# Taking two attention accumulators out of PSUM: one VectorE copy of 576 columns against one copy each by VectorE and ScalarE

## What is computed

```python
q_pool = q.reshape(B, H, S // 2, 2, D).mean(axis=3)
scores = scale * np.matmul(q_pool, k.transpose(0, 1, 3, 2))
attn = np.exp(scores - max(scores)); attn = attn / (sum(attn) + 1e-09)
x = np.matmul(attn, v)                       # -> (2304, 512)
h = x @ w_in;  x = (h * sigmoid(h)) @ w_out          # d_ff 2048
a = x @ w1; b = x @ w2; out = ((a * b) @ w3) @ w_out2
```

## Time and profile before

| | us |
|---|---|
| median of 3 runs | 1280.03 |
| lowest and highest | 1279.23, 1280.61 |
| the profiled execution | 1280.76 |
| its span, first to last instruction | 1278.6 |

### The profile page before, as it was taken

One profiled execution on the slowest core, in us unless ns is written; L12 is line 12 of the kernel. 1 busy time (PEld: TensorE's weight loads), 2 busy tenths in 40 slices (PEclk: granted clock), 3 DMA queues, 4 the chain that ended last, 5 costly groups with the idle time before them and its releaser, 6 DMA issues.

```text
span 1278.6 us, 26209 instructions
## 1 busy us (share of the span) xinstructions
PE 1268.6 (99%) x10968; PEld 1148.6 (90%) x10968; DVE 601.3 (47%) x895; ACT 587.6 (46%) x1065; POOL 378.1 (30%) x321
## 2 busy tenths in 40 slices
PE   8999999999999999999999999999999999999998
PEld 7999999999999999888888888888988888888888
DVE  6778877777787778723212121111155222222222
ACT  3777777777777777833222222222245212121111
POOL 5577777777777776210000000000000000000000
PEclk9999999999999999999999999999999999999999
DMA  4222222222222211021000000001062000000001
GB/s 143 66 75 73 66 73 72 74 76 75 75 75 75 75 57 38 27 68 50 9 1 1 1 1 1 1 1 50 1 207 74 1 26 8 10 24 1 33 8 42
DMA packets 26005, 58.59 MB, mean 46 GB/s; under 512 B 7200, under 2 KB 8736, under 8 KB 25888
## 3 DMA queue, kind: packets, MB, share of 16 engines
q1 hardware_dynamic: 25888, 56.91, 13.4%
HBM read 52.04 MB, written 4.79 MB: 44 GB/s over the span
## 4 chain that ended last, share of the span: by engine, by line
PE 97%; DVE 2%; DMA 0%; ACT 0%; issue 0%; DVEq 0%; ACTq 0%
PE psum L957 19%; PE psum L958 19%; PE psum L959 19%; PE psum L1035 18%; PE psum L974 10%; PE psum L1010 9%; PE psum L1012 3%; DVE mx L745 1%; PE psum L985 1%; DMA qraw<-in_qT 0%; DVE pL L780 0%; ACT pH L566 0%; PE psum L1045 0%; ACT tmpB L559 0%; ACT pF L574 0%
## 5 line engine op out<-in xcount | busy, mean ns | idle before, releaser
L745 DVE TENSOR_REDUCE mx<-psum 128x2 f32<-128x768 f32 x240 | 229.0, 958 | 85.3 <-PE psum L974 82.1
L566 ACT ACTIVATE pH<-psum 128x576 fp32r<-128x576 f32 x288 | 188.5, 655 | 133.9 <-PE psum L1012 129.1
L471 POOL TENSOR_TENSOR pL<-pF,pH 128x576 fp32r<-128x576 f32 x120 | 170.2, 1428 | 111.6 <-ACT pF L574 111.4
L888 DVE TENSOR_TENSOR gL<-gF,gH 128x512 fp32r<-128x512 f32 (+1 forms) x80 | 51.1, 639 | 310.2 <-ACT gH L647 310.2
L1035 PE MATMUL psum<-pH,vH 64*128 64x288 f32 x1152 | 180.5, 295 | 0.9 <-ACT tmpB L559 0.5
L1035 PE MATMUL psum<-pL,vH 64*128 64x288 f32 x1152 | 178.6, 292 | 0.8 <-DVE pL L780 0.8
L1035 PE MATMUL psum<-pH,vL 64*128 64x288 f32 x1152 | 178.5, 292 | 0.0
L644 ACT ACTIVATE gF<-psum 128x512 f32<-128x512 f32 (+1 forms) x80 | 44.4, 555 | 269.9 <-PE psum L959 269.9
L935 DVE TENSOR_TENSOR pr<-aS,psum 128x512 f32<-128x512 f32 (+1 forms) x40 | 25.4, 635 | 200.2 <-ACT aS L716 200.2
L1035 PEld LDWEIGHTS psum<-pH,vH 64*128 64x128 f32 x1152 | 117.0, 185 | 2.4 <-PE psum L1035 1.6
L957 PE MATMUL psum<-gH,woH 128*128 128x512 f32 (+1 forms) x320 | 117.9, 368 | 0.0
(11 more groups left out here) (104 smaller groups left out, 2762.5 us busy)
## 6 DMA issues: line engine op xcount, KB each, us to landing
vraw<-in_v SPq DMA_DIRECT2D x16, 576.0 KB, 4.5
qraw<-in_qT SPq DMA_DIRECT2D x15, 576.0 KB, 5.5
kraw<-in_kT SPq DMA_DIRECT2D x15, 576.0 KB, 3.7
rsums<-recips SPq DMA_DIRECT2D x32, 144.0 KB, 3.0
wstage<-in_w_in SPq DMA_DIRECT2D x16, 256.0 KB, 4.1
fstage<-in_w3T SPq DMA_DIRECT2D x8, 512.0 KB, 4.4
w12stage<-in_w SPq DMA_DIRECT2D x8, 512.0 KB, 4.7
outT<-oS SPq DMA_DIRECT2D x4, 1024.0 KB, 4.2
```

What stands on the lines that cost most here:

```text
L471: pool.tensor_tensor(pL[r][:], pF[SLOT[n]][:], pH[r][:].bitcast(F32), ALU.subtract).then_inc(pL_pool, 1)
L566: act.activation(pH[r][:], scores, ACT.Exp, scale=SCALE).then_inc(pH_ready, 1)
L745: dve.tensor_reduce(mx[:, qt, :, kb], bank[:, :, 0:KW], AX.X, ALU.max).then_inc(max_taken, 1)
L888: dve.tensor_tensor(gL[r][:, w], gF[:, w], gH[r][:, w].bitcast(F32), ALU.subtract).then_inc(gL_ready, 1)
```

## The change

One VectorE instruction copies both accumulators, 2 x 288 = 576 columns from two banks, at VectorE's old place in the order; ScalarE's copies are gone. A tensor `outs` with room for both heads takes the place of `tmpA` and `tmpB`, in the same bytes of SBUF. `o_taken` counts one for each half.

```diff
-        tmpA, tmpB = [None, sb("tmpA1", [2, HALF])], [None, sb("tmpB1", [2, HALF])]
+        outs = [None, sb("outs1", [2, 2, HALF])]
...
-                sp.wait_ge(o_taken, 4 * (p + 1))
-                for tmp, row, into in ((tmpA[p % 2], D, 0), (tmpB[p % 2], 0, 1)):
+                sp.wait_ge(o_taken, 2 * (p + 1))
+                for hd, row, into in ((0, D, 0), (1, 0, 1)):
...
-            def take_o(p, a):
-
-                act.wait_ge(pv_done, 2 * (UNITS * p + NC * (a + 1)))
-                need(act, normalized, 2 * (p - 1))
-                act.copy(tmpB[p % 2][:, a, :], obank[1]).then_inc(o_taken, 1)
-
...
-                if n % NC == 1 and n > NC:
-                    take_o((n - NC) // UNITS, (n - NC) // NC % 2)
...
                 dve.wait_ge(pv_done, 2 * (UNITS * p + NC * (a + 1)))
                 need(dve, normalized, 2 * (p - 1))
-                dve.tensor_copy(tmpA[p % 2][:, a, :], obank[0]).then_inc(o_taken, 1)
-                if p == PAIRS - 1 and a == 1:
-                    dve.tensor_copy(tmpB[p % 2][:, a, :], obank[1]).then_inc(o_taken, 1)
+                dve.tensor_copy(outs[p % 2][:, :, a, :], psum[:, 6:8, 0:HALF]).then_inc(o_taken, 1)
...
-                        need(pe, o_taken, 2 * (2 * p + a))
+                        need(pe, o_taken, 2 * p + a)
```

More of the change, by code:

```diff
@@ L102, in block_kernel @@
         with ExitStack() as st:
-            tmpA[0], tmpB[0] = sb("tmpA0", [2, HALF], F32, st), sb("tmpB0", [2, HALF], F32, st)
+            outs[0] = sb("outs0", [2, 2, HALF], F32, st)
             kraw = sb("kraw", [S], F32, st)
@@ L348, in pack_sums @@
             def pack_sums(p):
-                sp.wait_ge(o_taken, 4 * (p + 1))
-                for tmp, row, into in ((tmpA[p % 2], D, 0), (tmpB[p % 2], 0, 1)):
+                sp.wait_ge(o_taken, 2 * (p + 1))
+                for hd, row, into in ((0, D, 0), (1, 0, 1)):
                     sp.dma_start(packed[own(into), :],
-                                 tmp[row:row + 1, :, :].rearrange("o a b -> o (a b)").rearrange("o (a b) -> o a b", a=D)
+                                 outs[p % 2][row:row + 1, hd, :, :].rearrange("o a b -> o (a b)").rearrange("o (a b) -> o a b", a=D)
                                  ).then_inc(sums_packed, 16)
@@ L483, in normalize @@
                 need(pool, *before)
-                rows_of, tmp = own(hd), (tmpA, tmpB)[hd][p % 2]
-                pool.tensor_tensor(x_pair(p)[rows_of, :], tmp[rows_of, :, :].rearrange("p a b -> p (a b)"),
+                rows_of = own(hd)
+                pool.tensor_tensor(x_pair(p)[rows_of, :], outs[p % 2][rows_of, hd, :, :].rearrange("p a b -> p (a b)"),
                                    rsums[rows_of, :], ALU.mult).then_inc(normalized, 1)
```

## The result

| | median | lowest to highest | profiled execution | its span |
|---|---|---|---|---|
| before | 1280.03 | 1279.19 to 1280.62 (17 runs) | 1280.76 | 1278.6 |
| after | 1282.58 | 1281.96 to 1284.01 (17 runs) | 1283.09 | 1281.0 |

The ratio is 1.0022, 95% interval 1.0016 to 1.0029: the changed kernel takes 2.55 us longer, 0.20%. The forecast was 1283.5, with a range of 1280.9 to 1286.6. One of the eleven timed runs of cut192 took 3242.76 us, a slow one whose cause is not known, and its ratio leaves it out.

The account below looks back on a forecast made before the run. TensorE, busy for 99% of the span, was taken to bound the kernel. Boundaries 3.9 us and last pair -0.4 gave +3.5 on 1280.03: 1283.5 us, own range 1282.1 to 1285.0, stated range 1280.9 to 1286.6.

Parts of the forecast that it names:

- The copy: VectorE's 576-column copy out of two PSUM banks: takes 0.755 us and starts when the old one did.
- second value for the copy: From the Trainium skill's page: 725 ns for 576 columns, 0.03 us less at each of 29 boundaries, sum +2.6 us.
- Rival 3: Faster: copy ends after 0.6 us, TensorE waits for nothing and keeps the relief; -2.7 us, 1277.3; chance 0.05.
- the cover: TensorE's work hiding the copies: at mid-pair they end by 174.74, its last score starts at 174.89; said to be gone.
- The loss at a boundary: TensorE's net lateness at each wait for the copy: 0.14 us at 15 boundaries, 0.13 at 14; together 3.9 us.
- second head's lag: Behind such a wait, the second head's matmul follows the first's by some 0.03 us more, which later groups keep.
- The relief: Scores behind a boundary: without ScalarE's copy `pF` starts sooner and a small stall goes, 0.05 or 0.04 us back.
- Rival 1: The item's reduction behind the copy starts later and also delays TensorE: +6.7 us, 1286.7; chance 0.13.
- 0.06 us gap: Between the old copy's end (174.67) and the reduction (174.73): read as the reduction waiting for its item's scores.
- Rival 2: TensorE loses only its first group's slip, weights' loads catch up: 0.03 us a boundary, +0.5 us, 1280.5; chance 0.20.
- The last pair: +0.1 us at u = 2, -0.5 at u = 11 from earlier `pF`, perhaps ahead of GpSimd: -0.4, between -1.1 and -0.2.

Follow-up runs that it names:

- cut192: The changed kernel with its one copy cut to 192 columns a head, the rest filled once at the start: 1278.11 us against 1279.66, ratio 0.9988.
- cut240: The changed kernel with its one copy cut to 240 columns a head, the rest filled once at the start: 1280.46 us, ratio 1.0005.
- act_dummy: The changed kernel with ScalarE's copy back in its old place, into a tile nobody reads: 1283.24 us against 1279.66, ratio 1.0029.
- extra_dve: The changed kernel with one more VectorE fill between the copy and the reduction: 1288.36 us against 1279.43, ratio 1.0073.
- after_again: The changed kernel, unchanged, run once more in a later series: 1282.48 us against 1279.43, ratio 1.0024.
- no_act: The kernel before without ScalarE's copy, the second head's accumulator left out: 1278.37 us against 1279.66, ratio 0.9988.

## Why the prediction was right, and where it was not

**The copy** was put at 0.755 us, took 0.757, and starts where the old one did. TensorE's second group follows 0.35 us behind its end, as read from the earlier trace rows. These carry the sign and most of the size. The second value for the copy that the prediction gives, 0.03 us shorter, fell; that its sum of +2.6 is next to the measured +2.55 is luck. Rival 3 (faster) fell with the copy's length; its condition was right, though: it needed a copy of 0.6 us, and the cover is 0.59 by cut192 and cut240. cut192, which meets it, is 1.55 us faster than the kernel before and not 2.7: the 1.3 of the boundaries came (14 x 0.094), of the last pair's 1.2 to 1.5 only 0.7.

**The loss at a boundary** was put at 0.14 and 0.13 us, a pair at 0.27. Measured: 0.229 and 0.239 a pair. The term that was mis-sized is the second head's lag, 0.02 to 0.03 us a boundary. Without it the prediction's own sums are 0.12 + 0.10 = 0.22. Rows do last 0.33 us behind the wait (0.32 for the first scores, at 175.64), as they did at the end of a pair before, but the starts of the rows follow each other as they did, 0.13 us apart, and these make the time. The 29 boundaries cost 14 x 0.229 + 0.15 = 3.4 us (the 0.15 is the boundary between copies 29 and 30); the forecast is 3.9 and its lower bound 3.2.

**The relief** was a wrong step with a right number. "Without the copy `pF` starts in its place" and the stall goes: the stall does go, but act_dummy shows that it goes with `pF` as late as ever. The reason given for it was ScalarE; the cause is TensorE's own lateness. The consequence is not small for other changes: a loss of 0.17 us at one wait swallows a stall of 0.05 just behind it, so that losses in a row don't add up, and the relief on the second engine is not what makes the loss smaller here. ScalarE's busy time was to fall by 12.2 us and fell by 7.8: the 12.2 are 31 copies at their recorded length, but a copy and the `pF` behind it start only 0.28 us apart in the earlier trace rows, which makes 8.7.

**Rival 1** (the reduction counts too) fell: the reduction starts at 174.93, 0.09 us ahead of the copy's end, and from the copy's start to it are 0.67 us. In the kernel before and in cut192 it starts 0.52 us behind the copy's start, with copies of 0.458 and 0.557 us, so there it does not wait for the copy's end; the prediction's reading of the 0.06 us gap fits that. The prediction also says that the trace does not agree with "The DRAIN you can't avoid" of the Trainium skill's page "VectorE: DVE Perf Modes". That section says as well that a next operation which isn't held starts earlier, so a start 0.09 us ahead of the end doesn't contradict it. extra_dve shows its condition to be right all the same: what delays the reduction by more than some 0.07 us costs TensorE nearly in full.

**Rival 2** (no more than can be told from no change) had +0.5 us, and the measured +2.55 is clear of it: its interval goes from 0.16% to 0.29%, that is from 2.0 to 3.7 us. The 2.6 us that the prediction took for what a measurement tells were too coarse for 17 runs, and by them alone the result would count as no change. Its mechanism was wrong. It has the weights' loads catch up, with 0.03 us a boundary; the boundaries cost 0.115.

**The last pair** was put at -0.4 us, +0.1 at u = 2 and -0.5 behind u = 11. Measured from the 30th copy to the 31st +0.14, and from there to the feed-forward -0.22 in one profile and -1.18 in the other. The 0.28 us that `pF` was to gain did come: from the copy's start to `pL` it is 0.82 us in after (530.18, then 531.00) and 1.13 before (527.52, then 528.65). But GpSimd's instruction, which comes when a DMA lands, does not stand still meanwhile: it starts 0.73 us behind that copy's start and not 0.96. So `pL` lost the race by 0.09 us as it had by 0.17. This is the step that failed in this term: the prediction held GpSimd's start fixed at 528.48 and let `pF` decide, and what decides is when the DMA lands. In after_again it landed so much sooner that GpSimd's first instruction was over (531.06) when `pL` began. What the prediction describes, `pL` ahead of GpSimd's first, is seen in no_act and cut240 (by 0.11 and 0.15 us), with 12.83 us for the stretch in both, 0.83 less than before. To take a value between the outcomes was a choice that the runs neither bear out nor refute, since they don't show how often each comes.

**The sum.** 3.4 + 0.14 - 0.22 = +3.3 us is what the profile's attention part shows (+3.28), or +2.5 with the race won, against +3.5. The medians differ by 2.55, and by 3.05 in after_again. The race and the start of the kernel, both about 1 us, may be what lies between; the runs don't show it.

## What to carry to other kernels

Where TensorE is busy for all of a stretch, the views of busy time and waits show neither a cover of 0.1 us nor the waits that take its place. Measure them from the starts on either side of one boundary, write down the end of the wait, the cover and the lead-in (here 0.35 us from a producer's end to the second group), and multiply by the count. Merging two copies of two engines into one makes the one that is waited for longer (757 ns for 458 here), and it costs nothing only while it fits under the cover: 0.59 us here. Small losses one behind another on the same engine need not sum: here the first took in the next.

## What the runs showed that was not expected

**The start.** The first unit starts at 23.39 us before and at 22.54 after, although the change does nothing there. TensorE's first 32 matmuls, whose products nobody reads, and the first ones on data, in the timelines of before and of after:

```profile
1.12 4.21 PE L1045 MATMUL psum<-pH 64*128 64x288 f32 x32 [1.12 <-POOL pH L490]
...
6.77 0.52 PE L974 MATMUL psum<-kL,qH 64*128 64x384 f32 x2
7.09 0.52 PE L974 MATMUL psum<-kH,qL 64*128 64x384 f32 x2
```

```profile
1.12 3.73 PE L1035 MATMUL psum<-pH 64*128 64x288 f32 x32 [1.12 <-POOL pH L490]
...
6.46 0.33 PE L964 MATMUL psum<-kL,qH 64*128 64x384 f32 x2
6.63 0.34 PE L964 MATMUL psum<-kH,qL 64*128 64x384 f32 x2
```

Groups of 384 columns are 0.32 us apart before and 0.17 after: 1.2 GHz and 2.4 GHz, though the granted clock stands as 1.00 in both. Before, this lasts until 9.33 us, and the first unit is 0.85 us later for it. The 32 matmuls start at 1.12 us in all ten profiles and take 4.21 us in the slow starts, and 3.71 to 4.09 in five of the six fast ones, where the speed rises before they are over; in cut240 they take 4.21 too, and its matmuls on data are fast all the same. In the ten profiles the slow start stands with the four profiles of programs that have `tmpA` and `tmpB` (first unit at 23.2 to 23.4 us), the fast one with the six of programs with `outs` (22.4 to 22.7), four of which do the same work ahead of the first copy. That may be the program or chance. The timed runs of the kernel before don't tell: they fill the stretch from 1279.19 to 1280.62, and its two profiled executions, 1280.76 and 1280.59, lie above all timed ones of their series. It stays open. It is also why the spans should not be compared alone here: the change costs 3.28 us in the attention part of its profile, and 0.85 of it are hidden by a start that it does not cause in any way that was found.

**Starts ahead of ends.** The reduction behind the copy starts 0.09 us ahead of its recorded end (174.93 against 175.02), as in the earlier trace rows, and so does the one behind the extra instruction (176.88 against 176.97), but that instruction itself starts 0.01 us behind the copy's end (176.67 against 176.66). The overlap is a matter of the pair of instructions, not of the engine alone.
